# First attention tiles: k and the first query tile loaded as a piece of their own, and the second tile's scores in four other PSUM banks

## The chip, the cores and the metric

The kernel runs on one core of a Trainium2 chip. The metric is the device time of one execution in microseconds (us). The median of three runs of the kernel before is 998.66 us (998.6 to 999.17).

## The reference

Three layers follow one another, all in fp32. The change touches the first.

```python
# 1: attention, batch 4, 8 heads, 576 positions, head size 64
scores = scale * q @ k.T                       # scale = 64 ** -0.5
thresh = max(scores, axis=-1) - tau            # tau = 0.02
scores = where(scores >= thresh, scores, -1e9)
attn = softmax(scores)                         # sum + 1e-9 below the line
x = attn @ v                                   # -> 2304 tokens x 512
# 2: mixture of experts: 8 experts, 512 -> 1024 -> 512, one chosen for each token
#    (gate logits + a term by the token's modality), relu, times the gate's probability
# 3: x @ w_in (512 x 2048), h * tanh(softplus(h)), @ w_out (2048 x 512)
```

## The kernel before, in words

**Tiles.** Attention goes over 16 pairs of heads (batch and two heads). A pair has 576 query positions, cut into four tiles of 128 positions, each with two heads, and a fifth tile with the last 64 positions of both heads. So there are 80 tiles, numbered n. TT = 5 is the number of tiles of a pair, QT = 4.

**One tile's way.** PE computes the scores of both heads (L373 to L376; the fifth tile L379 and L380) into PSUM: head 0 in banks 0 and 1 (`a_bank`), head 1 in banks 2 and 3 (`b_bank`). DVE copies each head to SBUF with the scale and takes the row's minimum of the negated scores (L600, `copied`). ACT makes the exponential (L497, `exp_done`). POOL adds the margin from tau to the row's minimum (`find_limit`, L294, `limited`). DVE multiplies the exponentials by the comparison with that limit and sums the row (L613, `prob_done`). PE transposes the result (`turn`, L388, L392, L397) into banks 4, 5 and 6, ACT copies it to SBUF (L506, L507), PE multiplies with v (`pv`, L416, L419) and then with a matrix `wx` made of an identity and gate weights (`rows_out`, L443), and DVE normalises (L641).

**Order on each engine.** All queues are written out by hand, in one loop over c on each engine, with semaphores between the engines:
- PE: first the wait for the constants (L359), then for each c: scores(c), pv(c-3), turn(c-2), rows_out(c-3). At the start that is scores(0), scores(1), scores(2), turn(0), scores(3), pv(0), turn(1), rows_out(0), scores(4).
- DVE: six small operations on tau (L576 to L581), then for each c: copy of tile c (both heads), masking of tile c-1 (both heads), normalising of tile c-3.
- ACT: exponential of head 0 of tile c, output copy of c-3, exponential of head 1 of tile c, copies of the transposed tile c-2.
- POOL: constants (L255 to L275), then the wait for three small tables (`small_in`, L278), then 16 copies that build `wx` (L285, L286), and then find_limit(0), find_limit(1) and so on.

**Waits of scores(n).** It waits for the pair's q and k when a pair begins (L365), and from n = 1 on until every copy of the tile before is done (L367), because all tiles use the same four banks. scores(2) thus waits for both copies of tile 1.

**Loads.** They are issued by SP (`sync`): tau; then q and k of pair 0, v of pair 0, q and k of pair 1, v of pair 1; then gate weights (wg), modality terms (mb) and modality ids (modi), on which `small_in` counts. A pair's qk array is [128, 1280] fp32 (640 KB): 576 columns of q, 576 of k, and 128 for the fifth tile's queries. Later pairs are loaded when the buffers are read out (L231, L233).

Of the kernel before, what the change touches and what calls it, by code (L numbers as in the profile page):

```python
# [13 lines left out]
ALU = mybir.AluOpType  # L14
# [7 lines left out]
P = 128  # L22
B, H, S, D = 4, 8, 576, 64
# [9 lines left out]
HALF = S // 2  # L33
# [22 lines left out]
ALL_CONSTS = 17  # L56
# [27 lines left out]
def units(n):  # L84

    return TPP * (n // TT) + 2 * (n % TT)
# [7 lines left out]
def attention_phase(nc, t, io):  # L94
# [73 lines left out]
    consts = sem("consts")  # L168
    tau_in = sem("tau_in")
    small_in = sem("small_in")  # L170
    qk_in = [sem("qk_in0"), sem("qk_in1")]
    v_in = [sem("v_in0"), sem("v_in1")]
    wx_done = sem("wx_done")
# [31 lines left out]
    OUT0 = 512 - 4 * HW  # L205
    row_bank = psum[:, 7, OUT0:512]

    def q_of(u):
        return qk[:, u, 0:S]

    def k_of(u):
        return qk[:, u, S:2 * S]

    def sync(sp):
        sp.dma_start(taub[:], io["tau"].partition_broadcast(P)).then_inc(tau_in, 16)
        for u in range(2):
            sp.dma_start(qk[:, u], io["qk"][u]).then_inc(qk_in[u], 16)
            sp.dma_start(vsb[:, u], io["v"][u]).then_inc(v_in[u], 16)
        sp.dma_start(wg[:], io["w_gate"]).then_inc(small_in, 16)
        sp.dma_start(mb[:].rearrange("p m e -> p (m e)"),  # L220
                     io["mbias"].partition_broadcast(P)).then_inc(small_in, 16)
        sp.dma_start(modi[:].rearrange("p t c -> p (t c)"), io["mod"]).then_inc(small_in, 16)
        for n in range(2, PAIRS):
            u = n % 2
            if n == CLEAR_AT:
                sp.wait_ge(lead_ready, 1)
                for i in range(EARLY):
                    row = sp.value_load(tab["early"][0:1, i:i + 1], min_val=i * P, max_val=(E - 1) * CAP + i * P)
                    sp.dma_start(io["xs"][bass.ds(row, P), :], t["zrow"][:]).then_inc(cleared, 16)
            sp.wait_ge(scores_done, TT * (n - 1))  # L230
            sp.dma_start(qk[:, u], io["qk"][n]).then_inc(qk_in[u], 16)  # L231
            sp.wait_ge(pv_done, TT * (n - 1))
            sp.dma_start(vsb[:, u], io["v"][n]).then_inc(v_in[u], 16)  # L233
        sp.sem_inc(y_stored, 16 * YRING)
        sp.wait_ge(cleared, 16 * EARLY)
        sp.wait_ge(scattered, 16 * TT * (B - 1))
        for i in range(EARLY):
            row = sp.value_load(tab["early"][0:1, i:i + 1], min_val=i * P, max_val=(E - 1) * CAP + i * P)
            early["load_row"](sp, i, row)
        sp.wait_ge(ends_known, 1)  # L240
        sp.wait_ge(t["x_in"], 16 * EARLY)
        for e in range(E):
            row = sp.value_load(tab["ends"][0:1, e:e + 1], min_val=e * CAP, max_val=e * CAP + N)
            sp.dma_start(io["xs"][bass.ds(row, P), :], t["zrow"][:]).then_inc(t["padded"], 16)
        sp.wait_ge(tables, 1)
        sp.wait_ge(scattered, 16 * TT * B)
        sp.wait_ge(t["padded"], 16 * E)
        early["load_x"](sp, EARLY)
        for i in range(EARLY):
            sp.wait_ge(y_out, i + 1)  # L250
            sp.wait_ge(y_stored, 16 * (i + YRING))
            sp.dma_start(io["ys"][i * P:(i + 1) * P, :], t["ysb"][:, i % YRING, :]).then_inc(y_stored, 16)
# [103 lines left out]
            scatter(B - 1, tt)  # L356

    def tensor(pe):
        pe.wait_ge(consts, ALL_CONSTS)  # L359

        def scores(n):
            p, tt = divmod(n, TT)
            u = p % 2
            if tt == 0:
                pe.wait_ge(qk_in[u], 16 * (p // 2 + 1))  # L365
            if n >= 1:
                pe.wait_ge(copied, units(n))  # L367
            q, k = q_of(u), k_of(u)
            if tt < QT:
                cols = slice(tt * P, (tt + 1) * P)  # L370
                qa, qb = q[0:D, cols], q[D:P, cols]
                ka, kb = k[0:D], k[D:P]
                pe.matmul(a_bank[:, 0, :], qa, ka[:, 0:HALF], start=True, stop=True)  # L373
                pe.matmul(b_bank[:, 0, :], qb, kb[:, 0:HALF], start=True, stop=True)
                pe.matmul(a_bank[:, 1, :], qa, ka[:, HALF:S], start=True, stop=True)
                pe.matmul(b_bank[:, 1, :], qb, kb[:, HALF:S], start=True, stop=True).then_inc(scores_done, 1)  # L376
            else:
                qr = qk[:, u, 2 * S:]
                pe.matmul(a_bank[:, 0, :], qr, k[:, 0:HALF], start=True, stop=True)  # L379
                pe.matmul(a_bank[:, 1, :], qr, k[:, HALF:S], start=True, stop=True).then_inc(scores_done, 1)  # L380

        def turn(n):
            w, full = n % 3, n % TT < QT
            pe.wait_ge(prob_done, units(n) + 1)
            if n >= 1:
                pe.wait_ge(main_out, n)
            for j in range(QT):
                pe.transpose(turn_bank[:, 0, j * P:(j + 1) * P], prob[:, w, j * P:(j + 1) * P], ident[:])  # L388
            if full:
                pe.wait_ge(prob_done, units(n + 1))  # L390
                for j in range(QT):
                    pe.transpose(turn_bank[:, 1, j * P:(j + 1) * P],  # L392
                                 prob[:, w, S + REM + j * P:S + REM + (j + 1) * P], ident[:])
            if n >= 1:
                pe.wait_ge(rest_out, n)
            if full:
                pe.transpose(rest_bank, prob[:, w, QT * P:QT * P + P], ident[:]).then_inc(turned, 1)  # L397
            else:
                pe.transpose(rest_bank[0:REM, :], prob[:, w, QT * P:S], ident[:]).then_inc(turned, 1)
# [159 lines left out]
    def vector(dve):  # L559
# [33 lines left out]
        def copy_scores(n, h):  # L593
            w = n % 2
            if h == 0:
                dve.wait_ge(scores_done, n + 1)
                if n >= 2:
                    dve.wait_ge(prob_done, units(n - 1))
                    dve.wait_ge(limited, n - 1)
            dve.tensor_scalar(ssb[:, w, h * S:(h + 1) * S].rearrange("p (a q) -> p a q", a=2),  # L600
                              b_bank if h else a_bank, factor, BIG, ALU.mult, ALU.min,
                              accum_out=smin[:, w, h:h + 1]).then_inc(copied, 1)

        def probs(n, h):
# [946 lines left out]
def host_layout(q, k, v, tau, moe_modality_id, moe_w_gate, moe_modality_bias, moe_w1, moe_w2, moe2_w_in, moe2_w_out):  # L1551

    import numpy as np
    c = np.ascontiguousarray

    qT = q.reshape(PAIRS, 2, S, D).transpose(0, 1, 3, 2).reshape(PAIRS, P, S)
    kT = k.reshape(PAIRS, 2, S, D).transpose(0, 1, 3, 2).reshape(PAIRS, P, S)
    kT[:, D:P] = np.roll(kT[:, D:P], REM, axis=2)
    q_rest = np.zeros((PAIRS, P, P), q.dtype)
    q_rest[:, 0:D, 0:REM], q_rest[:, D:P, REM:P] = qT[:, 0:D, QT * P:], qT[:, D:P, QT * P:]  # L1560
    vp = v.reshape(PAIRS, 2, S, D)
    v_main = vp[:, :, :QT * P].reshape(PAIRS, 2, QT, P, D).transpose(0, 3, 1, 2, 4).reshape(PAIRS, P, 2 * QT * D)
    rest = vp[:, :, QT * P:]
    v_blocks, v_rest = np.zeros((PAIRS, P, P), v.dtype), np.zeros((PAIRS, P, P), v.dtype)
    v_blocks[:, 0:REM, 0:D], v_blocks[:, REM:P, D:P] = rest[:, 0], rest[:, 1]
    turned = np.roll(vp[:, 1], REM, axis=1)
    v_rest[:, 0:REM, 0:D], v_rest[:, 0:REM, D:P] = rest[:, 0], turned[:, QT * P:]
    v_turn = turned[:, :QT * P].reshape(PAIRS, QT, P, D).transpose(0, 2, 1, 3).reshape(PAIRS, P, QT * D)
    mod = np.zeros((B, TT * P), moe_modality_id.dtype)
    mod[:, :S] = moe_modality_id.reshape(B, S)  # L1570
    mod = mod.reshape(B, TT, P).transpose(2, 0, 1).reshape(P, B * TT)

    w1 = moe_w1.reshape(E, KT, P, F1).transpose(0, 2, 1, 3).reshape(E, P, WCOLS)
    w2 = moe_w2.reshape(E, FT1, P, DM).transpose(0, 2, 1, 3).reshape(E, P, WCOLS)
    w_out = moe2_w_out.reshape(FT2, P, DM).transpose(1, 0, 2).reshape(P, 2, WCOLS)
    wa = np.concatenate([w_out[None, :, 0], w1[::-1]])
    wb = np.concatenate([w_out[None, :, 1], w2[::-1]])
    return {"qk": c(np.concatenate([qT, kT, q_rest], axis=2)), "v": c(np.concatenate([v_main, v_blocks, v_rest, v_turn], axis=2)),
            "tau": c(np.reshape(tau, (1,))), "mod": c(mod), "w_gate": c(moe_w_gate),
            "mbias": c(moe_modality_bias.reshape(-1)), "wa": c(wa), "wb": c(wb), "w_in": c(moe2_w_in)}  # L1580

# [18 lines left out]
```

## Time and profile before

| | us |
|---|---|
| median of three runs | 998.66 |
| profiled execution, its own time | 998.59 |
| its span in the trace | 996.9 |
| PE busy | 964.4 |
| DVE busy | 675.2 |
| ACT busy | 503.5 |
| POOL busy | 484.3 |

The span is what the trace covers, from the first instruction to the last; the execution's own time is 1.7 us longer. PE is TensorE's matmuls, PEld its weight loads, DVE VectorE, ACT ScalarE, POOL GpSimd, SP the engine that issues most DMAs. Times in rows are counted from the span's start.

### The profile page before, as it was taken

What the parts mean: (1) busy time and instruction counts of PE and PEld (TensorE: products, weight loads), DVE (VectorE), ACT (ScalarE), POOL (GpSimd) and SP (SyncE); (2) the same over time, 40 slices, a digit from 0 to 9 for tenths busy, and PEclk for the clock granted to TensorE, in tenths of its full rate; (3) what the DMA queues carried; (4) which work ended last, traced back from release to release, by engine and by line L of the source; (5) the groups of instructions that cost most, each with busy time, mean ns of one, the idle gap of its engine ahead of it and who ended that gap; (6) DMA issues with size and microseconds to landing.
All of it is one profiled execution on the core that took longest, in us unless ns stands there. A gap on an engine that the chain in (4) does not pass through costs nothing.

```text
span 996.9 us, 17681 instructions
## 1 busy us (share of the span) xinstructions
PE 964.4 (97%) x6176; PEld 803.5 (81%) x6177; DVE 675.2 (68%) x1223; ACT 503.5 (51%) x971; POOL 484.3 (49%) x575
## 2 busy tenths in 40 slices
PE   6999999999998999999999989999999999999996
PEld 4777777777776878888887778988889889898995
DVE  5788888978885451111115489978878888888784
ACT  3656666666665242222225455555555545455552
POOL 3222225765432156400000066786786776777885
PEclk9999999999999999999999999999999999999999
DMA  2212227222111437311124300000100100000000
GB/s 99 73 49 70 76 84 267 101 73 90 64 68 54 161 110 274 100 45 45 44 75 150 142 32 1 33 33 1 33 32 1 33 32 1 33 1 1 33 1 32
DMA packets 21785, 65.85 MB, mean 66 GB/s; under 512 B 3536, under 2 KB 3536, under 8 KB 21456
## 3 DMA queue, kind: packets, MB, share of 16 engines
q1 hardware_dynamic: 14368, 39.90, 11.7%
q0 software_dynamic: 4896, 20.00, 5.6%
q10 hardware_dynamic: 2448, 5.01, 1.8%
q8 instruction: 42, 0.69, 0.3%
q14 instruction: 31, 0.25, 0.1%
HBM read 46.63 MB, written 18.27 MB: 65 GB/s over the span
## 4 chain that ended last, share of the span: by engine, by line
PE 85%; POOL 5%; DVE 4%; issue 3%; ACT 1%; DMA 0%; ACTq 0%; DVEq 0%; POOLq 0%; SPq 0%
PE psum L416 6%; PE psum L1302 5%; PE psum L1286 5%; PE psum L1288 5%; PE psum L1287 5%; PE psum L1304 5%; PE psum L1303 5%; PE psum L373 4%; PE psum L388 4%; PE psum L1000 3%; PE psum L973 3%; PE psum L1002 3%; PE psum L1001 3%; PE psum L975 3%; PE psum L974 3%
## 5 line engine op out<-in xcount | busy, mean ns | idle before, releaser
L1400 DVE RECIPROCAL rr<-rr 128x384 f32<-128x384 f32 x96 | 244.1, 2543 | 9.3 <-ACT rr L1348 9.3
L497 ACT ACTIVATE prob<-ssb,smin 128x576 f32<-128x576 f32 x144 | 111.6, 776 | 105.4 <-DVE ssb L600 105.4
L1236 POOL TENSOR_TENSOR uu<-uu,ex 128x384 f32<-128x384 f32 x96 | 97.2, 1013 | 105.0 <-ACT uu L1342 104.5
L600 DVE TENSOR_SCALAR_CACHE_REDUCE ssb<-psum,tauk 128x576 f32<-128x576 f32 x144 | 112.6, 816 | 47.1 <-PE psum L376 39.2
L1286 PE MATMUL psum<-x2T_hi,w_in_hi 128*128 128x384 f32 x384 | 131.0, 341 | 1.7 <-DVE x2T_lo L1418 1.7
L294 POOL TENSOR_TENSOR limit<-smin,margin 128x2 f32<-128x2 f32 (+1 forms) x80 | 57.6, 720 | 148.1 <-DVE ssb L600 147.7
L1288 PE MATMUL psum<-x2T_hi,w_in_lo 128*128 128x384 f32 x384 | 129.5, 337 | 0.0
L1287 PE MATMUL psum<-x2T_lo,w_in_hi 128*128 128x384 f32 x384 | 129.1, 336 | 0.0
L1052 DVE TENSOR_TENSOR hT_lo<-psum,hT_hi 128x512 fp32r<-128x512 f32 x38 | 26.3, 691 | 146.9 <-ACT hT_hi L1029 146.9
L1302 PE MATMUL psum<-w_hi,g_hi 128*128 128x512 f32 x288 | 114.8, 399 | 6.5 <-POOL g_lo L1247 6.5
L1304 PE MATMUL psum<-w_hi,g_lo 128*128 128x512 f32 x288 | 114.3, 397 | 0.0
L1303 PE MATMUL psum<-w_lo,g_hi 128*128 128x512 f32 x288 | 114.1, 396 | 0.0
L1242 POOL TENSOR_TENSOR rr<-uu,rr 128x384 f32<-128x384 f32 x96 | 97.8, 1018 | 29.6 <-DVE rr L1400 29.4
L613 DVE SCALAR_TENSOR_TENSOR prob<-ssb,limit,prob 128x576 f32<-128x576 f32 x144 | 112.0, 810 | 0.0
L1348 ACT ACTIVATE rr<-uu 128x384 f32<-128x384 f32 x96 | 50.5, 526 | 118.8 <-POOL uu L1236 118.8
L1247 POOL TENSOR_TENSOR g_lo<-gg,g_hi 128x384 fp32r<-128x384 f32 x96 | 99.6, 1037 | 1.6 <-ACT g_hi L1354 1.1
L1023 ACT ACTIVATE hid<-psum 128x512 f32<-128x512 f32 x38 | 22.7, 599 | 123.4 <-PE psum L975 123.4
L1339 ACT ACTIVATE ex<-ex 128x384 f32<-128x384 f32 x96 | 50.5, 526 | 63.0 <-DVE ex L1395 62.7
L1395 DVE TENSOR_SCALAR ex<-psum 128x384 f32<-128x384 f32 x96 | 52.9, 552 | 35.1 <-PE psum L1288 35.0
L1286 PEld LDWEIGHTS psum<-x2T_hi,w_in_hi 128*128 128x128 f32 x384 | 72.4, 189 | 5.1 <-issue 1.9
L416 PEld LDWEIGHTS psum<-pt,vsb 128*64 128x64 f32 x1024 | 54.6, 136 | 26.1 <-ACT pt L506 18.7
L1287 PEld LDWEIGHTS psum<-x2T_lo,w_in_hi 128*128 128x128 f32 x384 | 72.5, 189 | 3.4
(206 smaller groups left out, 2213.3 us busy)
## 6 DMA issues: line engine op xcount, KB each, us to landing
qk<-in_qk_dram SPq DMA_DIRECT2D x16, 640.0 KB, 4.1
vsb<-in_v_dram SPq DMA_DIRECT2D x16, 512.0 KB, 3.5
xrow<-xs ACTq DMA_DIRECT2D x17, 288.0 KB, 2.8
ys<-ysb SPq DMA_DIRECT2D x19, 257.0 KB, 3.1
stage<-in_w_in_dram POOLq DMA_DIRECT2D x16, 256.0 KB, 3.6
wa<-in_wa_dram SPq DMA_DIRECT2D x8, 512.0 KB, 6.8
wb<-in_wb_dram SPq DMA_DIRECT2D x8, 512.0 KB, 10.5
xs<-zrow SPq DMA_DIRECT2D x11, 288.0 KB, 2.4
```

The costliest lines, as they stand in the source:

```text
L416: pe.matmul(ot_bank[h * D:(h + 1) * D, :], vsb[:, u, (h * QT + j) * D:(h * QT + j + 1) * D], pt[:, w, (h * QT + j) * P:(h * QT + j + 1) * ...
L497: act.activation(prob[:, n % 3, cols], ssb[:, w, cols], ACT.Exp, bias=smin[:, w, h:h + 1], scale=-1.0).then_inc(exp_done, 1)
L600: dve.tensor_scalar(ssb[:, w, h * S:(h + 1) * S].rearrange("p (a q) -> p a q", a=2), b_bank if h else a_bank, factor, BIG, ALU.mult, ALU.m ...
L613: dve.scalar_tensor_tensor(out=prob[:, n % 3, cols], in0=ssb[:, w, cols], scalar=limit[:, w, h:h + 1], in1=prob[:, n % 3, cols], op0=ALU.i ...
L1247: pool.tensor_tensor(g_lo[:, n % 4], gg[:, n % 2], g_hi[:, n % 4].bitcast(F32), ALU.subtract).then_inc(g_lo_done, 1)
L1286: pe.matmul(bank_of(n), w_in_hi[:, k, cols], xT_hi[w][:, k], start=(k == 0), stop=False)
L1287: pe.matmul(bank_of(n), w_in_hi[:, k, cols], xT_lo[w][:, k], start=False, stop=False)
L1288: last = pe.matmul(bank_of(n), w_in_lo[:, k, cols], xT_hi[w][:, k], start=False, stop=(k == KT - 1))
L1302: pe.matmul(out_bank[j], g_hi[:, n % 4, q], w_out_hi[half][:, fh], start=(f == 0), stop=False)
L1303: pe.matmul(out_bank[j], g_hi[:, n % 4, q], w_out_lo[half][:, fh], start=False, stop=False)
L1304: return pe.matmul(out_bank[j], g_lo[:, n % 4, q], w_out_hi[half][:, fh], start=False, stop=(f == FT2 - 1))
L1400: dve.reciprocal(rr[:, n % 4], rr[:, n % 4]).then_inc(r_done, 1)
```

## The change

The layout of a pair's qk array becomes k, q, fifth tile's queries, so that k and the first 128 query columns lie side by side: 704 columns, 352 KB. For pair 0 they are loaded by a DMA of their own with the semaphore `first_in`, issued ahead of tau; the rest of pair 0's array (288 KB) follows tau. SP then waits until both have landed before it issues v of pair 0, and everything that stands behind it. scores(0) waits for the first piece alone, scores(1) for the rest. PE's wait for the constants moves to the first transpose. Tile 1's scores go to banks 4 to 7, so scores(1) doesn't wait for the copies of tile 0; the wait for copies begins with n = 2, and DVE reads tile 1 from there.

```diff
+    first_in = sem("first_in")
...
+    def banks(n):
+
+        return (psum[:, 4:6, 0:HALF], psum[:, 6:8, 0:HALF]) if n == 1 else (a_bank, b_bank)
+
+    def k_of(u):
+        return qk[:, u, 0:S]
+
     def q_of(u):
-        return qk[:, u, 0:S]
-
-    def k_of(u):
         return qk[:, u, S:2 * S]
 
     def sync(sp):
+        sp.dma_start(qk[:, 0, 0:S + P], io["qk"][0, :, 0:S + P]).then_inc(first_in, 16)
         sp.dma_start(taub[:], io["tau"].partition_broadcast(P)).then_inc(tau_in, 16)
-        for u in range(2):
-            sp.dma_start(qk[:, u], io["qk"][u]).then_inc(qk_in[u], 16)
-            sp.dma_start(vsb[:, u], io["v"][u]).then_inc(v_in[u], 16)
+        sp.dma_start(qk[:, 0, S + P:], io["qk"][0, :, S + P:]).then_inc(qk_in[0], 16)
+        sp.wait_ge(first_in, 16)
+        sp.wait_ge(qk_in[0], 16)
+        sp.dma_start(vsb[:, 0], io["v"][0]).then_inc(v_in[0], 16)
+        sp.dma_start(qk[:, 1], io["qk"][1]).then_inc(qk_in[1], 16)
+        sp.dma_start(vsb[:, 1], io["v"][1]).then_inc(v_in[1], 16)
         sp.dma_start(wg[:], io["w_gate"]).then_inc(small_in, 16)
...
     def tensor(pe):
-        pe.wait_ge(consts, ALL_CONSTS)
-
         def scores(n):
             p, tt = divmod(n, TT)
             u = p % 2
-            if tt == 0:
+            if n == 0:
+                pe.wait_ge(first_in, 16)
+            elif tt == 0 or n == 1:
                 pe.wait_ge(qk_in[u], 16 * (p // 2 + 1))
-            if n >= 1:
+            if n >= 2:
                 pe.wait_ge(copied, units(n))
+            a_bank, b_bank = banks(n)
             q, k = q_of(u), k_of(u)
...
         def turn(n):
             w, full = n % 3, n % TT < QT
+            if n == 0:
+                pe.wait_ge(consts, ALL_CONSTS)
             pe.wait_ge(prob_done, units(n) + 1)
...
             dve.tensor_scalar(ssb[:, w, h * S:(h + 1) * S].rearrange("p (a q) -> p a q", a=2),
-                              b_bank if h else a_bank, factor, BIG, ALU.mult, ALU.min,
+                              banks(n)[h], factor, BIG, ALU.mult, ALU.min,
                               accum_out=smin[:, w, h:h + 1]).then_inc(copied, 1)
...
-    return {"qk": c(np.concatenate([qT, kT, q_rest], axis=2)), "v": c(np.concatenate([v_main, v_blocks, v_rest, v_turn], axis=2)),
+    return {"qk": c(np.concatenate([kT, qT, q_rest], axis=2)), "v": c(np.concatenate([v_main, v_blocks, v_rest, v_turn], axis=2)),
```

## Rows read from the trace of the kernel before

**Rows 1.** The page: an engine's busy time, share and instructions; the chain's shares.
```profile
PE 964.4 (97%) x6176; PEld 803.5 (81%) x6177; DVE 675.2 (68%) x1223; ACT 503.5 (51%) x971; POOL 484.3 (49%) x575
...
PE 85%; POOL 5%; DVE 4%; issue 3%; ACT 1%; DMA 0%; ACTq 0%; DVEq 0%; POOLq 0%; SPq 0%
```

**Rows 2.** Busy by stretch: PE, PEld, DVE, ACT, POOL, granted clock, DMA share, GB/s.
```profile
100.00:200.00 100.00, 99.51 (x962) 77.14 (x962) 84.48 (x261) 64.97 (x128) 45.26 (x65) 1.00 0.37 131
...
6.00:8.00 2.00, 2.00 (x8) 1.11 (x8) 0.00 (x0) 0.00 (x0) 0.00 (x0) 1.00 1.03 421
```

**Rows 3.** Timeline of SP's issues: start us, us, then what is issued.
```profile
0.91 0.39 SPq L215 DMA_DIRECT2D taub<-in_tau_dram  x1
...
1.35 0.42 SPq L217 DMA_DIRECT2D qk<-in_qk_dram  x1
...
1.82 0.42 SPq L218 DMA_DIRECT2D vsb<-in_v_dram  x1
...
4.73 0.47 SPq L222 DMA_DIRECT2D modi<-in_mod_dram  x1
```

**Rows 4.** Single DMAs, issued at 1.82, 4.73, 23.75 and 36.1: KB, us to landing.
```profile
vsb<-in_v_dram SPq DMA_DIRECT2D x1, 512.0 KB, 5.2
...
modi<-in_mod_dram SPq DMA_DIRECT2D x1, 20.0 KB, 5.7
...
qk<-in_qk_dram SPq DMA_DIRECT2D x1, 640.0 KB, 4.1
...
vsb<-in_v_dram SPq DMA_DIRECT2D x1, 512.0 KB, 3.8
```

**Rows 5.** Timeline of PE's first weight loads: start us, us; in brackets idle before, releaser.
```profile
5.84 0.28 PEld L373 LDWEIGHTS psum<-qk 64*128 64x128 f32 x1 [5.53 <-POOL evalid L275]
...
9.82 0.28 PEld L373 LDWEIGHTS psum<-qk 64*128 64x128 f32 x1 [2.48 <-DVE ssb L600]
```

**Rows 6.** Timeline of DVE, POOL and ACT: start us, us, what; idle before in brackets.
```profile
4.67 0.15 DVE L581 COPY margin<-margin 128x1 f32<-128x1 f32 x1
...
10.59 0.23 POOL L285 COPY wx<-ident 64x64 f32<-64x64 f32 x1 [5.33 <-DMA modi<-in_mod_dram]
...
13.31 0.20 POOL L294 TENSOR_TENSOR limit<-smin,margin 128x2 f32<-128x2 f32 x1
...
13.64 0.82 DVE L613 SCALAR_TENSOR_TENSOR prob<-ssb,limit,prob 128x576 f32<-128x576 f32 x1
...
14.38 0.82 DVE L613 SCALAR_TENSOR_TENSOR prob<-ssb,limit,prob 128x576 f32<-128x576 f32 x1
...
18.40 0.99 ACT L506 COPY pt<-psum 128x1024 f32<-128x1024 f32 x1
```

**Rows 7.** The chain that ended last, first 22 us: start us, us on it, what.
```profile
1.35 4.39 DMA qk<-in_qk_dram
...
5.87 0.82 PE psum L373
...
8.20 1.58 DVE ssb L600 x4
...
13.78 0.84 PE psum L373
...
16.07 1.04 PE psum L388 x4
...
18.18 0.78 PE psum L373
...
20.08 1.02 PE psum L416 x16
21.10 0.42 PE psum L419 x2
```

**Rows 8.** Timeline of PE during scores(3): start us, us.
```profile
18.75 0.68 PE L373 MATMUL psum<-qk 64*128 64x288 f32 x1
...
19.67 0.40 PE L375 MATMUL psum<-qk 64*128 64x288 f32 x1
```

## The prediction

> **What bounds the kernel now.** I read the page's engine totals and the shares of the chain of waits first: PE is busy for 97% of the span, and 85% of the chain that ended last is PE [rows 1]. Then the table by stretches of 100 us: in 100 to 200 us PE is busy for 99.51 of 100 us while DVE, the next engine, has 84.48 [rows 2]. So PE's instruction queue sets the end: an idle or slow microsecond that PE loses or wins at the start arrives at the end, unless a later wait depends on absolute time. I found none: the later loads and waits follow from scores_done, pv_done and the like, so they move with PE.
>
> Then I read only the first 24 us, as a chain and as a timeline, since the diff touches nothing later. I call an attention tile's matmuls scores(n), its PSUM copies copy(n) (L600), its masking probs(n) (L613), its transposes turn(n), its value product pv(n). PE's order is scores(0), scores(1), scores(2), turn(0), scores(3), pv(0), turn(1). PE starts at 5.84, and its idle time lies before scores(1) and scores(2): each waits until DVE's copy has emptied the only two score buffers (scores at 9.82 after copy(0) from 8.20, scores(2) at 13.78) [rows 5, 7]. From 13.78 on PE is practically never idle. What ends before turn(0) is another chain: SP's small tables (the third is modi) land, POOL builds wx with 16 copies, only then comes limit(0) at 13.31, and probs(0) at 13.64 needs it [rows 3, 4, 6]. In the kernel before that chain is just in time, because DVE leaves copy(1) at about 13.6 too. That is what decides this change.
>
> **The change part by part.**
>
> *k and the first query tile first.* The piece is 704 of 1280 columns, 352 KB of 640. It is issued first, so at 0.91 (where tau's was) and not at 1.35; 640 KB took 4.39 us from a cold start [rows 7] and 4.1 us alone later [rows 4]. Together with the rest it thus lands at 0.91 + 4.1 to 0.91 + 4.39, 5.0 to 5.3. The other 288 KB at 421 GB/s [rows 2] are 0.70 us, so the first piece lands at 4.3 to 4.6; I take 4.5, and 5.2 for the rest. PE's wait for the constants moves to turn(0), where it costs nothing: it was met by 5.84, ten us earlier [rows 5]. tau goes behind the first piece. DVE's six small operations on it ended at 4.82, the last starting at 4.67, with tau issued at 0.91 [rows 3, 6]; issued 0.44 later and behind 352 KB (0.85 us of data at 421 GB/s), they end at about 6.1, before scores(0) ends at 6.9. That cover is 0.8 us.
>
> *Four other banks for scores(1).* scores(0) runs from 4.6 and takes 2.3 us (5.87 to copy's 8.20) [rows 5, 7], to 6.9. scores(1) follows at once, to 9.1. DVE copies tile 0 from 6.95 to 8.5 and tile 1 from 9.1 to 10.7 (1.58 us each [rows 7]). scores(2) can start at 10.7 where it started at 13.78. So on PE alone the change takes 3.1 us from the path, and adds no instruction on an engine. If that held to the end, it would be 995.5.
>
> *What SP does for it.* SP now waits for both pieces before it issues v0, qk1, v1, wg, mb and modi. v0's issue goes from 1.82 to about 5.25 (5.05 to 5.35), and behind it on SP's queue stand the three small tables that POOL waits for. Before, v0 landed at 1.82 + 5.2 = 7.02 and modi at 4.73 + 5.7 = 10.43, 3.41 us later, the queue running full [rows 3, 4]. A v load issued into an empty queue takes 3.8 us [rows 4]: v0 lands at 9.05 and modi at 9.05 + 3.41 = 12.46. Issue time is no bound: modi's issue came 2.91 us after v0's, so it falls at 8.2. From below: 1.66 MB at 421 GB/s (3.95) behind the 2.55 us that a 3.8 us v load spends on other than its 1.25 us of data, and 0.4 for the small ones, from 5.05: 11.95. From above: modi landed 9.08 us after qk0's issue; less the 1.56 us that qk0's own 640 KB take at 421 GB/s that is 7.5, from 5.35: 12.85. I take 12.45: the small tables come 2.0 us later than before.
>
> The Trainium skill, DMA: Bandwidth & Descriptors, on the cost of a DMA, gives about 2.0 us fixed beside bytes at 436 GB/s; by that v0 would take 3.2 us where the row has 3.8, the tables would land near 11.85, and the sum below would come out 0.6 lower. I keep to the row.
>
> *What that does to the path.* From modi's landing to probs(0)'s start were 13.64 - 10.43 = 3.21 us (16 copies, limit(0), semaphores) [rows 6]. That distance now is not hidden by copy(1), which ended at 10.7: DVE sits idle until 12.45 + 3.2 = 15.65. Behind the waiting probs(0) on DVE stand copy(2) and probs(1), and scores(3) waits for copy(2). probs(0) takes 2 x 0.74 and copy(2) 1.58 us [rows 6, 7], so scores(3) can start at 15.65 + 3.1 = 18.75, a little after turn(0) is through: it starts at 15.65 + 0.85 and takes 2.1 (16.07 to 18.18 [rows 7]), 18.6. Before, scores(3) started at 18.18 on the chain. **All three microseconds of scores are eaten, and 0.6 is lost.** The bounds 11.95 and 12.85 for the tables give 18.25 and 19.15, so 0.1 to 1.0 lost.
>
> *TensorE's rate.* The same 64x288 matmul takes 0.68 us until 18.75 and 0.40 from 19.67 on, and the transposes L388 0.26 each in the first group (1.04 for four); the granted clock column says 1.00, which would be 2.4 GHz, from the start on, so I go by the durations [rows 2, 7, 8]. The short ones came in the middle of scores(3), with PE at work without a pause since 13.78. In the changed kernel PE stands idle from 13.0 to 16.5, so its uninterrupted work begins 2.7 us later, and turn(0) and scores(3) are then probably both wholly slow. scores(3) costs 2.29 us slow (13.78 to 16.07) where it cost 1.90 [rows 7]: +0.4. pv(0) costs 1.44 us fast [rows 7]; wholly slow it would cost up to twice that, +1.4 (estimate). Bounds: 0 and +1.8, and +2.8 if turn(1) cost the 2.1 us of turn(0) and not half of it. I take 0.4 + 0.3: the rate rises a little after scores(3), within the first half of pv(0), where before it rose within scores(3). Nor can a fast scores(3) win much: pv(0) waits for ACT's copy of tile 0 (L506, 0.99 us [rows 6]), in front of which ACT has the exponential of tile 2's second head, which needs copy(2). By 18.75 + 0.8 (estimate, from DVE's 0.82 us for the same 128x576) + 1.0 pv(0) can't start before 20.6, against 20.08 [rows 7].
>
> The Trainium skill, TensorE: Matmul & The Clock Gate, on the HAM clock gate, says that sustained matmuls release the clock and an idle stretch throttles it again. By that the two tiles back to back from 4.6 to 9.1 may make the rate rise before 10 us. This trace has no such pair to show it; if the rate also outlived the idle 3.5 us, the sum would be the +0.5 of pv(0)'s wait for ACT, and if it did not, the sum below.
>
> **Sum:** 0.6 (scores(3) later) + 0.7 (rate) = 1.3 us. The profiled execution had 998.59 us (span 996.9 and 1.7 around it), 0.07 under the median of 998.66. So 999.9 us. About 0.2%, 2.0 us, is what a measurement of this kernel tells from no change; the forecast lies inside it.
>
> **The rivals.**
>
> A, slower: the rate stays low through pv(0) and turn(1). 0.6 + 0.4 + 1.4 + 1.0 = 3.4 us, 1002.0. For it: PE has its longest pause right before. Against: before, the rate rose within the first tile after turn(0), and here two tiles back to back precede. It decides at about 22.9 us, where a slow pv(0) would end (18.75 + 2.3 + 1.9): if the matmuls are still long there, the kernel is slower by about 0.2% or more.
>
> B, a little faster: the tables don't come later, since the rings are emptied faster than I reckon or SP's waits end sooner. With modi at 10.43, probs(0) starts at 13.65 and scores(3) at 16.8, a gain of 1.4, of which a slow scores(3) and pv(0) give back 0.4 to 1.8: 997.6 to 999.0, at 998.0. Against it: the same bytes begin 3.4 us later on SP's queue, behind a fixed part that is paid twice.
>
> C, faster in full: POOL isn't what probs(0) waits for, and the 3.1 us of scores reach the end: 995.5. For it: the trace shows no wait of DVE for POOL before probs(0). Against: it had no room for one, since copy(1) and limit(0) ended together, and POOL's program order puts the 16 copies ahead of limit(0).
>
> D, the first piece gains nothing, because both pieces' packets are mixed on the rings and land together at 5.3. Then scores(0) starts at 5.4 and copy(1) ends at 11.5, still long before 15.65: the end is that of the forecast, 999.9.
>
> **Chances.** Forecast with D, from 0 to +2.0 us: 0.68. A and what lies above +2.0: 0.17. B, without its part beyond -2.0: 0.09. C, with that part: 0.06. The range takes in the forecast's bounds and most of B and A's lower half: 998.0 to 1001.8. Faster by over 0.2% 0.06, within 0.77, slower 0.17.
>
> **What would show it.** Right: first scores matmul at about 4.6; scores(1) without a gap, ending near 9; scores(2) near 10.7; modi landing near 12.5 and POOL's first wx copy right after it; DVE idle 5 us before probs(0), which starts near 15.7; PE idle 3.5 us before turn(0); scores(3) near 18.8; long matmuls to between 21 and 22 us. From 26 us on, the same pace per tile. Wrong: a wx copy before 11, probs(0) before 14.5, or scores(3) before 17.5; or another stall in a later stage that grows or goes with the shift.

## The result, and the profile after

| | before | changed |
|---|---|---|
| median of 20 runs, us | 998.57 | 1001.06 |
| lowest to highest, us | 997.94 to 999.77 | 999.17 to 1001.86 |
| profiled execution, us | 998.59 | 1001.05 |
| its span, us | 996.9 | 999.4 |

The ratio is 1.0023, with a 95% interval of 1.0016 to 1.003: the changed kernel is 2.5 us slower, 1.6 to 3.0 by the interval. That is inside the predicted range and above the predicted 999.9. The forecast called it most likely within 0.2%; the median came out just above that line, and the interval holds the line.

The page of the changed kernel, the lines that answer to [rows 1]. PE's busy time has hardly moved (964.4 before). That sum hides two things of opposite sign, matmuls that ran faster and others that ran slower than before, so the page alone does not say where the 2.5 us are:

```profile
span 999.4 us, 17683 instructions
...
PE 964.6 (97%) x6176; PEld 804.3 (80%) x6177; DVE 675.3 (68%) x1223; ACT 503.4 (50%) x971; POOL 483.7 (48%) x575
```

The timeline of the changed kernel's first 20 us, in order of the start (start us, us, engine, what; in brackets idle before and what ended it). These lines answer to [rows 3, 5, 6]; L383 to L386 are the scores, L612 the copies, L625 the masking:

```profile
4.03 0.85 PE L383 MATMUL psum<-qk 64*128 64x288 f32 x1 [4.03 <-DMA qk<-in_qk_dram]
...
5.51 0.33 SPq L225 DMA_DIRECT2D vsb<-in_v_dram  x1
...
7.98 0.51 SPq L231 DMA_DIRECT2D modi<-in_mod_dram  x1
...
9.91 0.51 PE L383 MATMUL psum<-qk 64*128 64x288 f32 x1 [1.67 <-DVE ssb L612]
...
12.69 0.23 POOL L294 COPY wx<-ident 64x64 f32<-64x64 f32 x1 [7.43 <-DMA modi<-in_mod_dram]
...
15.72 0.82 DVE L625 SCALAR_TENSOR_TENSOR prob<-ssb,limit,prob 128x576 f32<-128x576 f32 x1 [5.86 <-POOL limit L303]
...
16.69 1.09 PE L400 MATMUL psum<-ident,prob 128*128 128x128 f32 x4 [5.54 <-DVE prob L625]
...
19.01 0.84 PE L383 MATMUL psum<-qk 64*128 64x288 f32 x1 [0.17 <-DVE ssb L612]
```

The reader is to see one line above all: DVE's masking of tile 0 sat idle for 5.86 us, and what ended it is POOL's limit. In [rows 6] the same instruction had no idle time in brackets. Everything that the new banks and the early piece won until 9.91 (scores(2) began at 13.78 before) was spent there. The wait runs back through POOL's copies to modi, which SP now issues at 7.98 and not at 4.73.

The chain of waits of the changed kernel around scores(3) and pv(0), to be read beside [rows 7] (start us, us on it, what):

```profile
19.01 0.84 PE psum L383
...
21.30 1.39 PE psum L428 x16
22.70 0.42 PE psum L431 x2
23.11 0.44 PE psum L400 x4
```

scores(3) is 0.83 later than before (18.18), pv(0) 1.22 (20.08), turn(1) 1.59 (it began at 21.10 + 0.42 = 21.52 [rows 7]).

**Where the other 0.9 us are.** I set the same instructions of both traces side by side, on ACT's queue, and looked at how much later each starts. From 23 us to 567 us they are 1.56 to 1.61 later (but for 18 near 387 and 399 us, which are 1.0 to 1.3 later and delay nothing behind them); at 592 us it is 2.29, from 612 us to the end 2.43 to 2.48. So the start gave 1.6 us, and 0.9 us came at one place, at 585 to 592 us. There, in both kernels, PE stands 3.9 us idle between the third layer's first up products and its first down product, and the granted clock falls. The stretches (PE busy and instructions, granted clock, DMA share, GB/s), first of the changed kernel, then of the one before:

```profile
584.00:586.62 2.62, 0.00 (x1) 0.74 0.00 0
586.62:592.00 5.38, 5.38 (x14) 0.50 0.00 0
592.00:594.00 2.00, 2.00 (x12) 0.99 0.04 8
```

```profile
584.00:586.00 2.00, 0.93 (x4) 1.00 0.00 0
586.00:589.40 3.40, 3.40 (x11) 0.53 0.00 0
589.40:592.00 2.60, 2.60 (x14) 0.95 0.03 6
```

At 0.50, 1.2 GHz, the 5.4 us of work of the changed kernel cost 2.7 us more than at 2.4 GHz; in the kernel before, 3.4 us at 0.53 cost 1.6 (worked out from the granted clock; the instructions' shift is 0.9). The same pause, another length of the slow stretch behind it. The clock's records in the two traces give the whole stretch at 1.2 GHz: 585.2 to 592.1 in the changed kernel, which begins 1.4 us before the pause ends, and 586.2 to 589.6 in the kernel before, which begins 1.2 us after it. The early pause has the same mark in the changed kernel:

```profile
9.90:10.97 1.07, 1.05 (x8) 1.00 1.02 418
10.97:16.60 5.63, 0.19 (x2) 0.57 0.13 23
16.60:21.30 4.70, 4.44 (x19) 0.50 0.00 0
21.30:22.95 1.65, 1.65 (x20) 0.78 0.00 0
```

scores(2) ran fast (1.05 us for eight matmuls), then PE stood idle for 5.5 us and did turn(0) and scores(3) at 1.2 GHz.

One trap in this column: these traces have no record of the clock for their first microseconds, and the column reads 1.00 where there is none. The records begin at 8.4 us in the changed kernel and at 19.6 in the kernel before, just where its matmuls turn from long to short (0.68 us at 18.75, 0.40 at 19.67 [rows 8]). So a 1.00 ahead of the first record, such as the one at 6 to 8 us [rows 2], says nothing on the rate; there the durations do.

### The profile page after: what moved, and what is told of

Its sections match the earlier page's. It is cut to its first block, busy times and chain, and to the rows that moved or that the text cites. A ratio compares the mean times of both kernels' runs of the same rounds, so it can differ in the third digit from the quotient of the medians.

```text
span 999.4 us, 17683 instructions
## 1 busy us (share of the span) xinstructions
PE 964.6 (97%) x6176; PEld 804.3 (80%) x6177; DVE 675.3 (68%) x1223; ACT 503.4 (50%) x971; POOL 483.7 (48%) x575
## 4 chain that ended last, share of the span: by engine, by line
PE 84%; POOL 5%; DVE 4%; issue 3%; ACT 1%; ACTq 0%; DVEq 0%; POOLq 0%
PE psum L428 7%; PE psum L1314 5%; PE psum L1300 5%; PE psum L1298 5%; PE psum L1299 5%; PE psum L1315 5%; PE psum L1316 5%; PE psum L383 4%; PE psum L400 4%; PE psum L1012 3%; PE psum L985 3%; PE psum L1014 3%; PE psum L1013 3%; PE psum L987 3%; PE psum L986 3%
## 5 line engine op out<-in xcount | busy, mean ns | idle before, releaser
L612 DVE TENSOR_SCALAR_CACHE_REDUCE ssb<-psum,tauk 128x576 f32<-128x576 f32 x144 | 112.6, 816 | 41.7 <-PE psum L386 32.6
L625 DVE SCALAR_TENSOR_TENSOR prob<-ssb,limit,prob 128x576 f32<-128x576 f32 x144 | 112.0, 810 | 5.9 <-POOL limit L303 5.9
## 6 DMA issues: line engine op xcount, KB each, us to landing
wb<-in_wb_dram SPq DMA_DIRECT2D x8, 512.0 KB, 10.7
```

Of the source, the lines that this page charges most:

```text
L625: dve.scalar_tensor_tensor(out=prob[:, n % 3, cols], in0=ssb[:, w, cols], scalar=limit[:, w, h:h + 1], in1=prob[:, n % 3, cols], op0=ALU.i ...
```

## The experiments

My theory after the result: (1) at the start, SP's waits push the small tables behind the v loads, and the chain tables, 16 copies, limit(0), probs(0) takes the path; (2) the pause that this gives PE costs about 0.8 us of rate on top; (3) the last 0.9 us are a longer slow stretch behind the pause at 585 us. Rivals: the banks themselves cost; the pause costs, wherever the tables land; the waits on the copies and not POOL hold probs(0). The kernels ran in three groups, each beside many runs of the kernel before (998.23, 998.48 and 998.58 us).

| label | what it is | us, median | ratio to before, 95% |
|---|---|---|---|
| e1_banks_only | before + other banks | 999.12 | 1.000, 0.9989 to 1.001 |
| e2_loads_only | changed, old banks | 1001.04 | 1.0019, 1.0006 to 1.0032 |
| e3_no_sp_waits | changed, no SP waits | 1000.01 | 1.0005, 0.9994 to 1.0016 |
| e4_limit_first | changed, two limits ahead of the wx copies | 993.94 | 0.9948, 0.9931 to 0.9964 |
| e5_tables_first | changed, tables ahead of SP's waits | 993.74 | 0.9945, 0.993 to 0.996 |
| e6_busy_start | changed, unused matmuls in the early pause | 999.76 | 1.0019, 1.0007 to 1.003 |
| e7_after_busy_late | changed, unused matmuls in the late pause | 999.17 | 1.0001, 0.9992 to 1.001 |
| e8_before_busy_late | before, unused matmuls in the late pause | 997.41 | 0.9984, 0.9976 to 0.9993 |
| e9_tables_and_limit | e4 and e5 together | 994.20 | 0.9946, 0.9934 to 0.9959 |
| e10_before_tables_first | before, tables behind q and k | 998.16 | 0.9994, 0.9985 to 1.0003 |
| e11_banks_tables_first | e10 + other banks | 996.36 | 0.9979, 0.9969 to 0.999 |
| e12_best_filled | e9 + e7's matmuls | 991.94 | 0.9932, 0.9919 to 0.9945 |

### The two halves of the change: e1 and e2

e1 is the kernel before with `banks(n)`, the wait for the copies from n = 2 on, and DVE's read from there. e2 is the changed kernel with:

```diff
-        return (psum[:, 4:6, 0:HALF], psum[:, 6:8, 0:HALF]) if n == 1 else (a_bank, b_bank)
+        return a_bank, b_bank
...
-            if n >= 2:
+            if n >= 1:
                 pe.wait_ge(copied, units(n))
```

> The kernel before with the four other banks for tile 1 and nothing else; loads as before. Theory (the chain small tables - 16 wx copies - limit(0) - probs(0) sets the path after scores(2)): modi lands at 10.4 as before, scores(1) runs from 8.2 without waiting, scores(2) from about 11.9, probs(0) still starts at 13.6, so scores(3) starts at about 16.8 where it was 18.1; 1.4 us won less 0 to 1.8 for TensorE's rate: 997.2 to 999.0. Rival (the loss of the whole change comes from the banks, by PSUM or by the pause that they open): 1000 or more.

> The changed kernel with tile 1's scores back in the first four banks, waiting for the copies of tile 0; loads as in the changed kernel. Theory: the loads carry the loss. modi lands at 12.5, probs(0) at 15.7, scores(3) at 19.0 although scores(2) ends only at 14.2: early shift against before 1.0 to 1.6, 999.6 to 1001.2, like the changed kernel. Rival (the banks carry it): no loss, about 998.6 or less.

The loads carry the loss (e2, 1.0019), the banks do not (e1, no difference). In e2's trace the tables came even later than forecast (the first wx copy at 13.13, scores(3) at 19.45 and not 19.0), while the rate rose within scores(3) as in the kernel before; it is 1.27 us late from 25 us on and loses nothing at the late pause. Its 12 runs fall into five of 999.3 to 999.8, the profiled one among them, and seven of 1000.8 to 1005.5. But e1 missed its forecast of 997.2 to 999.0 by a little, though its timing was as forecast: scores(3) starts 1.16 us earlier than before, at 17.02. The chain of e1:

```profile
17.02 0.84 PE psum L378
...
19.31 1.70 PE psum L421 x16
21.00 0.42 PE psum L424 x2
21.42 0.44 PE psum L393 x4
```

pv(0)'s first 16 matmuls take 1.70 us where they took 1.02 [rows 7], and scores(3) 2.29 and not 1.90: turn(1) starts 0.10 us earlier than before and no more. The rate has eaten the banks' 1.1 us, and at the late pause e1's trace loses another 1.1: it is 0.2 us ahead at 580 us and 0.9 behind at 600. In e1 too PE runs scores(2) fast and then pauses, and the granted clock is 0.50 from 14 to 20 us.

### SP's waits alone: e3

```diff
         sp.dma_start(qk[:, 0, S + P:], io["qk"][0, :, S + P:]).then_inc(qk_in[0], 16)
-        sp.wait_ge(first_in, 16)
-        sp.wait_ge(qk_in[0], 16)
         sp.dma_start(vsb[:, 0], io["v"][0]).then_inc(v_in[0], 16)
```

> The changed kernel without SP's two waits ahead of v of pair 0: the pieces and the banks stay. Theory: modi lands near 10.5, 2 us earlier, probs(0) at 13.7, scores(3) at 16.9; the first scores start a little later than 4.0 at most. 1.3 us won against before less 0 to 1.8 for the rate: 997.3 to 999.1. Rival (what costs is the rate alone, from PE's pause, wherever the tables land): the pause before turn(0) is still some 2.5 us, so 1000 or more.

A miss: 1000.0 and not 997.3 to 999.1. It is about 1 us below the changed kernel and not clearly apart from the one before. Two steps were too hopeful. The tables came earlier than in the changed kernel but not at 10.5:

```profile
11.44 0.23 POOL L292 COPY wx<-ident 64x64 f32<-64x64 f32 x1 [6.18 <-DMA modi<-in_mod_dram]
...
14.47 0.82 DVE L623 SCALAR_TENSOR_TENSOR prob<-ssb,limit,prob 128x576 f32<-128x576 f32 x1 [4.38 <-POOL limit L301]
```

The first wx copy is 0.85 us later than in the kernel before [rows 6]. Of that, 0.72 is there when modi is issued, at 5.45 and not 4.73 [rows 3]: SP has one more DMA to issue ahead of it, and its issues of wg, mb and modi take 0.65, 1.01 and 0.68 us where they took 0.54, 0.53 and 0.47. And pv(0)'s 16 matmuls took 1.90 us on the chain, all slow. Taking the waits out moves the tables and leaves the pause. The profiled execution of e3 is also its slowest (1001.96): there another 2.6 us are lost around a pause at 371 us. It lasts 2.71 us and not 1.46, and the granted clock is 0.81 from 371 to 375 us, where the kernel before has 1.00. This says nothing on the start: up to there e3 is 0.86 us late.

### The disputed link, cut at both ends: e4 and e5

e4 leaves the loads as they are and changes POOL's order:

```diff
-        pool.wait_ge(small_in, 48)
-        (the 16 wx copies)
...
         pool.wait_ge(coef_done, 1)
+        find_limit(0)
+        find_limit(1)
+        pool.wait_ge(small_in, 48)
+        (the 16 wx copies)
```

e5 leaves POOL's order and changes SP's:

```diff
         sp.dma_start(qk[:, 0, S + P:], io["qk"][0, :, S + P:]).then_inc(qk_in[0], 16)
+        (wg, mb and modi)
         sp.wait_ge(first_in, 16)
         sp.wait_ge(qk_in[0], 16)
...
-        (wg, mb and modi)
```

> The changed kernel with find_limit(0) and find_limit(1) on POOL ahead of the wait for the tables and the wx copies; modi still lands at 12.5. Theory: probs(0) starts at about 9.9, behind copy(1), copy(2) right behind it, scores(3) at about 13.5 to 14 and PE never idle for long from 9.9: 3.5 to 4.5 us won against before, 994.1 to 995.2. Rival (the late loads cost in another way, on v, qk1 or bandwidth): no better than 998.6. Rival (the copies' wait, not POOL, holds probs(0)): 1001.

> The changed kernel with the three small tables issued right behind the rest of pair 0's q and k, ahead of SP's two waits. Theory (what costs is that the tables stand behind v, qk1 and v1): modi lands by 7, POOL's copies end by 9.7, probs(0) starts at 9.9 behind copy(1), scores(3) at 12.5 to 13.5, 4 to 6 us before the kernel before: 992.5 to 995. Rival (POOL's order and not the tables' landing): the copies still hold probs(0) to 13 or more, 997 to 998.5.

Both came out as the theory has it (e4 even 0.2 us below its forecast), over 7 us faster than the changed kernel, and over 4 faster than the kernel before. These two settle the start. In e4 modi lands as late as in the changed kernel, but nothing on the path waits for it any more; in e5 POOL has the same order, but the tables are there. The timeline of e4:

```profile
8.00 0.20 POOL L304 TENSOR_TENSOR limit<-smin,margin 128x2 f32<-128x2 f32 x1 [2.75 <-DVE ssb L616]
...
9.21 0.82 DVE L629 SCALAR_TENSOR_TENSOR prob<-ssb,limit,prob 128x576 f32<-128x576 f32 x1
...
12.50 0.51 PE L387 MATMUL psum<-qk 64*128 64x288 f32 x1 [0.78 <-DVE ssb L616]
...
12.58 0.68 POOL L295 COPY wx<-ident 64x64 f32<-64x64 f32 x1 [2.50 <-DMA modi<-in_mod_dram]
```

And of e5:

```profile
6.22 0.23 POOL L294 COPY wx<-ident 64x64 f32<-64x64 f32 x1 [0.97 <-DMA modi<-in_mod_dram]
...
9.63 0.81 DVE L625 SCALAR_TENSOR_TENSOR prob<-ssb,limit,prob 128x576 f32<-128x576 f32 x1
...
12.92 0.51 PE L383 MATMUL psum<-qk 64*128 64x288 f32 x1 [0.78 <-DVE ssb L612]
```

The masking of tile 0 follows copy(1) without a wait, scores(3) starts at 12.5 and 12.9 and runs fast (0.51 and not 0.84 us for its first matmul). Once PE has begun there is no pause over 1.8 us at the start, so the win of the banks and the win of the rate come together.

### The rate at the start: e6

```diff
             if n == 0:
                 pe.wait_ge(consts, ALL_CONSTS)
+                (4 times tile 1's eight score matmuls, results unread)
             pe.wait_ge(prob_done, units(n) + 1)
```

> The changed kernel with four repeats of tile 1's score matmuls, whose results nobody reads, on PE between scores(2) and turn(0); all waits and loads stay. Theory (of the early shift of 1.6 us, 0.8 is the tables and 0.8 TensorE's rate after the pause): PE works until about 14.9, turn(0), scores(3) and pv(0) run at the short durations, scores(3) starts at 19.0 as before and pv(0) at 20.6 to 20.9: early shift 0.5 to 0.9, about 1000.2. Rival (the rate costs nothing, all is the tables): early shift 1.6, 1001. If the repeats themselves run slow they end at 18.6 and delay turn(0), 1001 to 1003.

The traces answer more sharply than the times. PE stays at work from 11.86 to 16.5, the matmuls are short from 13.2 on and stay so, scores(3) starts where it did (19.07), and the shift against the kernel before is 0.86 us from 100 us on, and not 1.59. So 0.7 us of the early loss was rate, as far as two single traces can tell: in e6's, scores(2) was still slow (0.84 us for its first matmul, at 9.78), so the two starts are not quite alike ahead of the added matmuls either. The chain of e6 also shows what holds pv(0) when the rate does not (L516 is ACT's exponential, L525 its copy of tile 0, L435 pv(0)):

```profile
18.32 0.76 ACT prob L516
19.08 0.66 issue
19.73 1.00 ACT pt L525
20.73 0.14 issue
20.87 1.09 PE psum L435 x16
```

That is the bound of 20.6 that the prediction set. By time e6 is 999.76, with six of its 11 runs at 999.3 to 999.8 and five at 1001.2 to 1003.8. The profiled one is of the first kind and lost nothing more at the late pause; what the others lost was not profiled.

### The late pause: e7 and e8

```diff
         def down(c, n):
...
+            if n == 0:
+                for i in range(16):
+                    pe.matmul(out_bank[0], xT_hi[0][:, 0, 0:P], w_in_hi[:, 0, 0:512], start=True, stop=True)
             pe.wait_ge(g_lo_done, g + 1)
```

> The changed kernel with 16 matmuls 128x512, whose results nobody reads, on PE in the pause before the third layer's first down product (at 582.5 to 586.6). Theory (0.9 us of the loss is a longer slow stretch of TensorE behind that pause, which both kernels have): the slow stretch at 586 to 592 goes, 2.5 us less than the changed kernel, about 998.5, and narrower spread. Rival (0.9 us comes from elsewhere): this kernel less the one before with the same 16 matmuls stays at 2.5 us.

> The kernel before with the same 16 matmuls in the same pause (581.0 to 585.1). Theory: the slow stretch at 586.2 to 589.4 goes, 1.6 us less than before, about 996.8; the changed kernel with the same filling is then 1.6 us slower and not 2.5. Rival: the difference stays 2.5, or the filling gives neither anything.

Both are some 0.6 us above the forecast, and their difference, 1.8, is near the forecast 1.6. With the late pause filled, the granted clock is 1.00 from 580 to 594 us in both, the kernel before gains 1.1 us and the changed one 1.9 (against its 1001.06, which is from another group), and the two are 999.17 - 997.41 = 1.8 us apart (same chip, same group) and not 2.5. By the times alone 1.8 and 2.5 are not clearly apart, since the intervals of the three ratios are 1.4 to 1.8 us wide. The traces decide it: on PE's queue e7 is 1.8 us behind e8 from 25 us on (2.11 and 0.30 behind the kernel before) and still 1.8 behind it at the end (1.00 behind and 0.81 ahead), where the changed kernel's lag grew by 0.9 at this pause. With the pause filled, nothing is added there. The spread agrees: the filled kernel before has all of its 11 runs within 997.12 to 997.86. The filled changed kernel still spreads over 998.17 to 1001.5; its profiled execution was 2.1 us late after pv(0), which was wholly slow, where the changed kernel's was 1.6 late. Up to there the two are the same program, so the start itself varies with the rate: in e7 scores(2) was slow too (0.85 us for its first matmul), and the rate first rose at 23.2 us. Its pv(0), as a stretch with the granted clock and as an instruction group, shows the trap of above, a 1.00 without a record:

```profile
21.20:23.10 1.90, 1.90 (x18) 1.00 0.00 0
...
21.20 1.97 PE L429 MATMUL psum<-pt,vsb 128*64 128x128 f32 x16
```

### What each part is worth once the tables are early: e9 to e12

> Both cures together: the changed kernel with the tables ahead of SP's waits and the first two limits ahead of POOL's copies. Theory: PE's own order bounds it from scores(2) on. POOL was hardly late with either cure alone (limit(2) waited about 1 us for the copies with the limits first, nothing waited with the tables first); so 0 to 1 us under either alone, 993.0 to 993.9. Rival (the two cures add up, 4 us each): 990.

> The kernel before with the three tables issued behind q and k of pair 0, ahead of v; no pieces, old banks. Theory: the tables were no bound before, since DVE left copy(1) at 13.6 when limit(0) came: nothing won from them alone, 998.0 to 998.7. Rival (the tables bound the kernel before as well): 1 us or more won, 997.5 or less.

> The kernel before with the four other banks and the tables behind q and k of pair 0; pair 0's q and k in one load, no waits of SP. Theory: of the 4.7 us that the changed kernel with early tables wins, the separate first piece gives what it lands earlier, 5.74 - 4.0 = 1.8 us less; so 995.0 to 996.5 here. Rival (the banks alone win it, the piece nothing): 993.7.

> The changed kernel with both cures and the 16 unused matmuls in the late pause: the version that the runs point to. Theory: the fillings' 1.1 to 1.9 us come on top of the cures' 4.7, 991.7 to 992.6. Rival (the late slow stretch is already gone once the start has moved): no less than with the two cures alone.

e9, both cures, is like either alone (994.2, 0.3 above the forecast's upper end): they cut the same link. e10 shows that the tables were no bound in the kernel before (0.9994, no difference), although its first wx copy comes 3.5 us earlier, at 7.08: the change made them one. In e11, banks and early tables with q and k in one load, 2.2 us are won (0.9979); e5 has the separate piece beside these and wins 4.7. Those 2.5 us more are about what scores(0) starts earlier, 6.08 against 3.89; in the two traces e11 is 3.1 us ahead of the kernel before from 25 us on and e5 5.3, which is the same 2.2:

```profile
6.08 0.82 PE L379 MATMUL psum<-qk 64*128 64x288 f32 x1 [6.08 <-DMA qk<-in_qk_dram]
```

e12 is the fastest of all, 991.94: e9's start and the filled late pause, 2.3 us below e9 and 0.68% below the kernel before. It has the early piece, the other banks, the tables ahead of v, the first limits ahead of POOL's copies, and PE kept at work in the pause at 580 us. Its five runs are few.

## Why the prediction was right, and what it missed

The direction and the range were right, and for the start the mechanism as well. The place of the total in the range is partly luck: 0.9 of the 2.5 us came from a stage that the prediction did not look at, and the range held them because it had been made wide for other reasons.

- *First piece.* Forecast to land at 4.5, first scores at 4.6; they came at 4.03, since 352 KB took 3.1 us to land and not 3.4 to 3.7. It changed nothing, as rival D said it would not.
- *Banks.* scores(2) forecast at 10.7, measured 9.91: earlier by the 0.6 us of the piece, and from scores(0)'s first matmul to copy(1) it was 4.3 us (4.03 to 8.30), not 4.5.
- *SP's waits.* v0's issue was forecast at 5.25 and came at 5.51, modi at 12.45 and its first copy at 12.69, probs(0) at 15.65 and came at 15.72, scores(3) at 18.75 and came at 19.01. The tables were to be 2.0 us late, by the row of a lone v load, and were 2.1 (the first copy at 12.69 and not 10.59); the Trainium skill's lower fixed cost (DMA: Bandwidth & Descriptors, which fits it for DMAs issued by GpSimd, and these are SP's) would have put them at 11.85, and the measurement sides with the row. e4 and e5 show that this link and no other holds the start. The term 0.6 measured 0.83.
- *The pause.* PE was to be idle for 3.5 us before turn(0); it was 5.5, because scores(2) began 0.8 earlier and ran fast, which the prediction had only as a possibility.
- *Rate at the start.* 0.4 for scores(3) and 0.3 for pv(0) were forecast; the traces have 2.29 - 1.90 = 0.39 and 1.39 - 1.02 = 0.37, and e6 gives 0.7 us back. The matmuls were short again within pv(0), at about 22 us. Rival A, slow through turn(1), did not come in this trace; e7's, the same program at the start, has half of it, pv(0) slow to its end (1.91 us on the chain) and turn(1) fast.
- The rule of the Trainium skill's page TensorE: Matmul & The Clock Gate, that sustained matmuls release the clock and an idle stretch throttles it again, is what the trace shows here: scores(2) was fast after the two tiles back to back (0.51 us for its first matmul), and the rate did not outlive the pause. It did not come out so in every execution: after the same two tiles scores(2) was slow in the traces of e6 and e7 (0.84 and 0.85).
- *The sum.* 1.3 forecast for the start, 1.59 measured. The lower bound for the tables, 11.95, has a slip: three loads of 512, 640 and 512 KB are 1.70 MB and not 1.66, so it is 12.05. Nothing hangs on it.
- *The step that failed* is the first: "an idle or slow microsecond that PE loses or wins at the start arrives at the end, unless a later wait depends on absolute time". No wait did, but TensorE's rate did. The pause at 581 us was in the profile of before, with its 0.53 behind it, and I looked at nothing after 24 us. A pause whose length is the same in both kernels was followed by 3.4 us of slow work in one and 5.4 in the other. That, and the 0.3 by which the start was short, put the total over 2.0 us, the forecast's line between no change and slower.

What stays open: why the late slow stretch is long in some executions and short in others. By the clock's records it lasted 6.8 us in the traces of the changed kernel, e1, e5, e9 and e11, which lost 0.9 to 1.2 us there against the kernel before, and 3.4 us in those of the kernel before, e2, e3, e4, e6 and e10, which lost nothing. This does not follow the size or the sign of the early shift (-5.2 us in e5, -5.7 in e4). It varies within one kernel as well, as far as the mean granted clock of runs without a trace can tell: of the 81 runs of the kernel before in the three groups, 60 have 0.996 or 0.997, as its profiled one, with medians of 998.0 to 998.5, and 16 have 0.994, as the traces with a long stretch and a fast start, with medians of 999.4 to 999.5. Nor is the chance the same for every kernel: one of e10's 11 runs has 0.994, and nine of e11's 12.

The changed kernel's 20 runs have 0.991 to 0.996 in the four fastest (999.2 to 999.9 us), 0.989 in nine, as the profiled one, and 0.994 in the seven slowest (1001.5 to 1001.9). The mean does not order them, and one reason is that it leaves out the slow time ahead of the first record. A start as late as e7's (2.1 us, no slow record) and a long late stretch (0.9) would give 998.6 + 3.0 = 1001.6 us and 0.994, which is where the seven lie. This is an estimate; none of the seven has a trace. If it holds, the long stretch is in 16 of the changed kernel's 20 runs and so more frequent than in the kernel before.

## What to carry to other kernels

Before loads are reordered, list every load behind the ones that are held back, down to the smallest, and follow who waits for each: here three tables of 44 KB, whose product wx PE first reads at 22 us, stood in front of a 0.2 us instruction on GpSimd's queue that the whole path needs. Work that becomes ready early is worth its time only when the next gate opens early as well; otherwise it turns into a pause, and a pause can cost twice on TensorE, once as idle time and once in the rate behind it. Here those of 3.9 and 5.5 us did; those of 1.7 and 1.8 us in e5 and e4 left the matmuls behind them short. Differences of a few microseconds should be read with every later TensorE pause of 3 to 4 us in view, since the slow stretch behind it alone made 0.9 of the 2.5 us here.

## What the runs showed of the hardware

- A pause of PE of the same 3.9 us was followed by slow matmuls for 3.4 us in one execution and for 5.4 in another; filling it with 16 unused 128x512 matmuls took the slow stretch away (granted clock 1.00 throughout) and gained 1.1 us in the kernel before and 1.9 in the changed one.
- The whole stretch at 1.2 GHz around that pause was 3.4 us in six traces and 6.8 in five. It began in the changed kernel before the pause was over, and in the kernel before 1.2 us after PE was at work again.
- The clock's record in a trace begins late: at 8.4 us in the changed kernel, 19.6 in the kernel before, 23.2 in e7. In the kernel before, e4, e6 and e7, where PE is at work at that moment, the matmuls turn short there. Ahead of it the column reads 1.00 while 64x288 matmuls take 0.68 us (0.40 later), and a run's mean clock leaves this slow time out.
- Two DMAs of 352 and 288 KB, issued 0.9 us apart, landed at 4.0 and 5.4, where one of 640 KB, issued between them, landed at 5.7: cutting the load in two advances the first part by 1.7 us and the whole by 0.3.
